# Reordered opening, moved addresses of x, and expert results scattered by token half in an attention + MoE kernel

## The reference

```
for t in range(S):                                    # attention, B=4 H=8 S=768 D=48
    y[t]  = r[t] @ (state + (u*k[t]) outer v[t])
    state = w * state + k[t] outer v[t]
h = x @ w_in;  x = (h * sigmoid(h)) @ w_out           # 384 -> 2048 -> 384
logits = x @ w_gate + modality_bias[modality_id]      # 8 experts
e = argmax(logits); p = softmax(logits)[e]
out = p * (relu(x @ w1[e]) @ w2[e])                   # 384 -> 1024 -> 384
```

## Time and profile before

| | us |
|---|---|
| three runs | 800.28, 800.82, 802.55; median 800.82 |
| profiled execution | 802.33, of which span 800.7 |
| PE busy | 748.7 (93%) |
| DVE, ACT, POOL busy | 503.0, 422.0, 228.3 |

### The profile page before, as it was taken

How to read it: one execution, slowest core, us unless ns; L and a number is a source line. 1 busy time by engine, 2 the same in 40 slices (tenths; PEclk the granted TensorE clock), 3 DMA queues, 4 the chain that set the end, 5 groups by cost and what they waited for, 6 DMA issues and landing times. The chain is left out here.

```text
span 800.7 us, 24974 instructions
## 1 busy us (share of the span) xinstructions
PE 748.7 (93%) x9894; PEld 728.6 (91%) x9894; DVE 503.0 (63%) x1349; ACT 422.0 (53%) x1076; POOL 228.3 (29%) x350
## 2 busy tenths in 40 slices
PE   3489999999999999999999999996989999999994
PEld 3478899999999999999999999996989999999994
DVE  7679765866576556656676657216856666556662
ACT  4476554545364545455554555435545665566552
POOL 4422221242224222322233212102415333323330
PEclk9599999999999999999999999998999999999998
DMA  8932221222222222122222210313576665665561
GB/s 318 377 134 74 63 99 53 88 73 95 74 95 74 94 76 93 57 82 69 95 74 94 75 58 2 118 82 118 193 163 239 235 234 197 227 248 213 213 223 55
DMA packets 24159, 104.94 MB, mean 131 GB/s; under 512 B 4411, under 2 KB 9800, under 8 KB 20482
## 3 DMA queue, kind: packets, MB, share of 16 engines
q1 hardware_dynamic: 19362, 93.34, 33.5%
q0 software_dynamic: 4704, 10.29, 3.8%
HBM read 93.90 MB, written 10.11 MB: 130 GB/s over the span
## 5 line engine op out<-in xcount | busy, mean ns | idle before, releaser
L635 ACT ACTIVATE g<-ps_h 128x256 f32<-128x256 f32 x192 | 73.9, 385 | 214.2 <-PE ps_h L1023 182.6
L1021 PE MATMUL ps_h<-x_hi,wi_hi 128*128 128x256 f32 x576 | 165.1, 287 | 8.5 <-DVE x_lo L806 7.7
L1022 PE MATMUL ps_h<-x_lo,wi_hi 128*128 128x256 f32 x576 | 162.7, 282 | 0.0
L1023 PE MATMUL ps_h<-x_hi,wi_lo 128*128 128x256 f32 x576 | 162.5, 282 | 0.0
L1038 PE MATMUL ps_o<-wo_hi,g_hi 128*128 128x392 f32 x384 | 135.4, 353 | 2.5 <-DVE g_lo L839 1.5
L1039 PE MATMUL ps_o<-wo_lo,g_hi 128*128 128x392 f32 x384 | 130.7, 340 | 0.0
L1040 PE MATMUL ps_o<-wo_hi,g_lo 128*128 128x392 f32 x384 | 130.4, 340 | 0.0
L839 DVE TENSOR_TENSOR g_lo<-g,g_hi 128x256 fp32r<-128x256 f32 x192 | 82.4, 432 | 71.2 <-ACT g_hi L628 69.3
L506 POOL TENSOR_TENSOR store<-store,up_half 128x256 f32<-128x256 f32 x44 | 33.8, 769 | 324.0 <-PE ps_y L1008 322.4
L1021 PEld LDWEIGHTS ps_h<-x_hi,wi_hi 128*128 128x128 f32 x576 | 108.9, 189 | 10.5 <-DVE x_lo L806 7.9
L1022 PEld LDWEIGHTS ps_h<-x_lo,wi_hi 128*128 128x128 f32 x576 | 109.1, 189 | 0.0
(11 more groups left out here) (199 smaller groups left out, 1528.3 us busy)
## 6 DMA issues: line engine op xcount, KB each, us to landing
store<-in_w SPq DMA_DIRECT2D x28, 1536.0 KB, 6.1
store<-in_quads SPq DMA_DIRECT2D x48, 704.0 KB, 4.7
x_rows<-rows SPq DMA_DIRECT2D x12, 384.0 KB, 3.1
woT_raw<-in_woT SPq DMA_DIRECT2D x4, 768.0 KB, 10.5
wi_raw<-in_wi SPq DMA_DIRECT2D x4, 768.0 KB, 10.3
wo_raw<-in_wo SPq DMA_DIRECT2D x4, 768.0 KB, 12.0
store<-x_rows,entries POOLq DMA_INDIRECT x26
out_rows<-y,entries_out POOLq DMA_INDIRECT x26
```

Of the source, the lines that this page charges most:

```text
L635: S.activation(g[:, F % 2, :], ps_h[F % 2][:, 0:ETOK], ACT.Silu).then_inc(g_made, 1)
L1021: T.matmul(out, hi, x_hi[:, t % 2, c, :], start=(c == 0), stop=False)
L1022: T.matmul(out, hi, x_lo[:, t % 2, c, :], start=False, stop=False)
L1023: last = T.matmul(out, lo, x_hi[:, t % 2, c, :], start=False, stop=(c == KC - 1))
```

## The change

In the opening: ACT does `first_states` right after `x_high(3)`, ahead of slot 0, and the splits of up chunks 4 and 5 too; in the slots the splits then run six ahead instead of four. DVE does `x_low(3)` ahead of `scale(4)` and `sum_bonus(4)`. An unused buffer of 336 fp32 words per partition stands ahead of `x_hi`, and `warm` moves behind `rows`; one of 248 words stands ahead of `xe_hi`. In the experts' block: PE does all down chunks of half 0, then those of half 1, with the turn at the same count of matmuls; ACT scales half 0 once `half_summed` says so, and half 1 at the end; POOL scatters each half on its own semaphore. Between tiles 1 and 2 POOL does `results_landed(1)` and `shift_entries(1)` ahead of the wait for the list entries. At the end SP waits for the landing of the results, and POOL does not.

```diff
@@ front_block, buffers
+        sb("x_place", [P, 336])
         x_hi = sb("x_hi", [P, 2, KC, ETOK], F32R)
         x_lo = sb("x_lo", [P, 2, KC, ETOK], F32R)
-        warm = sb("warm", [P, 4])
...
         rows = sb("rows", [P, 2, EB, W])
+        warm = sb("warm", [P, 4])
@@ ACT, opening and slots
             x_high(3)
+            first_states()
             wi_high(3)
+            wi_high(4)
+            wi_high(5)
...
-                if F == 0:
-                    first_states()
...
-                if F < FCH - 4:
-                    wi_high(F + 4)
+                if F < FCH - 6:
+                    wi_high(F + 6)
@@ DVE, opening and slots
             wi_low(2)
+            x_low(3)
             scale(4)
             sum_bonus(4)
-            x_low(3)
             wi_low(3)
+            wi_low(4)
+            wi_low(5)
...
-                if F < FCH - 4:
-                    wi_low(F + 4)
+                if F < FCH - 6:
+                    wi_low(F + 6)
@@ experts_block, buffers
+        sb("xe_place", [P, 248])
         xe_hi = sb("xe_hi", [P, KC, ETOK], F32R)
@@ SP, end
             sp.wait_ge(w2_in, 16 * tiles)
             sp.sem_inc(sp_passed, 1)
+            sp.wait_ge(y_out, 16 * EB * tiles)
+            sp.sem_inc(sp_passed, 1)
@@ POOL
             def results_out(j):
-                pool.wait_ge(y_made, j + 2)
-                pool.sem_inc(pool_passed, 1)
                 for i in range(EB):
+                    pool.wait_ge(y_half if i == 0 else y_made, j + 1 if i == 0 else j + 2)
+                    pool.sem_inc(pool_passed, 1)
...
+            results_landed(1)
+            shift_entries(1)
             tiles = tiles_with_tokens(pool)
             pool.wait_ge(listed, 16 * TB)
             load_entries(table, 3)
-            results_landed(1)
-            shift_entries(1)
...
             pool.wait_ge(entries_in, 16 * (tiles + 1))
-            results_landed(tiles)
+            pool.sem_inc(pool_passed, 1)
@@ ACT, end of a tile
                 x_high(j + 1)
+                act.wait_ge(half_summed, j + 1)
+                act.wait_ge(entries_kept, j + 1)
+                nc.scalar.activation(y[:, 0, :], ps_y[0][:, 0:DM], ACT.Copy, scale=entries_out[:, 0, 1:2].bitcast(F32)).then_inc(y_half, 1)
                 act.wait_ge(y_summed, j + 2)
-                act.wait_ge(entries_kept, j + 1)
-                for i in range(EB):
-                    last = nc.scalar.activation(y[:, i, :], ps_y[i][:, 0:DM], ACT.Copy, scale=entries_out[:, i, 1:2].bitcast(F32))
-                last.then_inc(y_made, 1)
+                nc.scalar.activation(y[:, 1, :], ps_y[1][:, 0:DM], ACT.Copy, scale=entries_out[:, 1, 1:2].bitcast(F32)).then_inc(y_made, 1)
@@ PE, down chunks
                 pe.wait_ge(y_made, j + 1)
-                for f in range(FCH):
-                    if f == (FCH - 2 if first else FCH // 2):
...
+                for i in range(EB):
+                    for f in range(FCH):
+                        if i == 1 and f == (FCH // 2 if first else 0):
...
-                last.then_inc(y_summed, 1)
+                    last.then_inc(half_summed if i == 0 else y_summed, 1)
```

More of the change, by code:

```diff
@@ L1179, in experts_block @@
         y_made = sem("y_made")
+        y_half = sem("y_half")
+        half_summed = sem("half_summed")
         y_out = sem("y_out")
@@ L1436, in tile @@
                 pe.wait_ge(y_made, j + 1)
-                for f in range(FCH):
-                    if f == (FCH - 2 if first else FCH // 2):
[L1439 to L1446, removed]
+                for i in range(EB):
+                    for f in range(FCH):
+                        if i == 1 and f == (FCH // 2 if first else 0):
+                            if first:
+                                pe.wait_ge(ranks_read, 1)
+                            pe.wait_ge(x_gathered, 16 * EB * (j + 1))
+                            turn()
+                        if i == 0:
+                            pe.wait_ge(h_lo_made, FCH * j + f + 1 + 4)
+                            if f % (FCH // PIECES) == 0:
+                                pe.wait_ge(w2_lo_made, PIECES * j + f // (FCH // PIECES) + 1)
                         hi, lo = (x[:, f, i * P:(i + 1) * P] for x in (h_hi, h_lo))
```

## The result

| | before | after |
|---|---|---|
| median of four runs, us | 800.55 (799.39 to 802.55) | 786.86 (786.45 to 787.36) |
| profiled execution, us | 802.33 | 786.88 |
| its span, us | 800.7 | 785.2 |
| PE busy, us | 748.7 | 742.9 |

The ratio is 0.9827, 95% interval 0.9806 to 0.9847: 13.7 us less, where 12.2 were forecast. The profiled execution of before lay 1.8 us above its median, so the two traces differ by more, 15.5 us.

A forecast was written before the change was run, and what follows sets the result against it. PE, busy 748.7 of 800.7 us, was taken as the bound: only its gaps and time per matmul count. Savings of 4.5 + 3.7 + 1.0 + 3.0 = 12.2 us gave 790.1 profiled, 788.6 median; range 780 to 796.

The forecast's parts named there:

- the likeliest case: Whole kernel: the forecast itself, all four terms come as summed, 788.6 us median; chance 0.43.
- Opening, 4.5 us: Opening: x_low(3) first, first_states and splits in ACT's idle time; 4.1 us plus half of an uncertain 0.8 saved.
- bounds of 2.5 and 6: Opening: 2.5 us saved if only the held-up x_low counts, nothing of DVE's idle time; 6 at most.
- The three moments named: Opening signs: PE's first up matmul at 33 us, slot 5's gate products near 49.4, DVE's 5.73 us gap gone.
- half of 0.8: Opening: splits done ahead leave DVE fewer wi_low pieces where it is full; half of an uncertain 0.8 us counted.
- Addresses, 3.7 us: Up matmuls: paddings shorten their spacing, dense to 117.8 ns (1.7 us), expert to 115.6 ns (2.0 us).
- POOL's order, 1.0 us: Expert tile 2: earlier copies remove PE's 2.43 us wait and half-speed stretch; 1.0 us saved, 3.7 saved to 1.5 lost.
- Late next is the gather: Expert tile 2: PE reaches the turn about 3.7 us earlier, near 604.3, and waits there for the gather instead.
- rival (e): SP's wait does not free POOL, and PE's wait for the gather costs a clock fall; 792.3 us, chance 0.04.
- `entries_kept` is made before: Expert tiles: ACT's new wait for half 0 holds up only its scaling, so halves cost nothing inside the tiles.
- Halves and SP's wait, 3.0 us: End: one activation and one scatter less, 1.8 us, and POOL's drain starting earlier, 1.2 us.
- rival (b): Up matmuls: addresses do nothing, 8.5 us saved in all, 792.3 us; chance 0.25.

The follow-up runs named there:

- e4_pool: Kernel before with only POOL's results_landed(1) and shift_entries(1) moved ahead of the wait for the list entries; 800.98 us, ratio 1.0010.
- e5_sp: Kernel before with only the end changed: SP waits for the landing of the results, POOL goes straight to its drain; 798.95 us, ratio 0.9983.
- e10_scan: Changed kernel with paddings of 368 and 312 words, plus 8 words ahead of g and 56 ahead of h_hi; 788.65 us.

## Why the prediction was right

786.86 us was measured, 788.6 forecast, and the likeliest case was the one that came. By the steps of the sum:

- **Opening, 4.5 us.** 5.1 measured alone, inside the bounds of 2.5 and 6. The three moments named came at 33.36 (33), 49.39 (near 49.4), and DVE's gap of 5.73 us shrank to 0.87 and 2.67, though it had been expected to go. Three details were off. The first product came 0.4 us later than the 32.95 of the sum, since x_low(3)'s three pieces took 2.30 us and not 1.95. DVE reached the end of `scale(4)` early enough for `scores` to follow the first up step at once (35.57), so the 0.7 us allowed for a wait there was not spent. And the splits ahead were worth 0.8 to 1.8 us, not half of 0.8.
- **Addresses, 3.7 us, called weakly founded.** 5.3 measured alone. That an address has a price, and the direction, came out as forecast, but not from the ground given: two speeds of one placement can't come from its address, and they recur in other traces with xe at 64. Each term was mis-sized: dense up gained 2.3 ns (1.0 taken), 3.9 us over 1728; expert up 0.8 (2.2 taken), 0.8 us over 936; and expert down 3.0 ns over 624 matmuls, 1.9 us, had no term. The prediction wrote that `h_hi` moves along, and asked no further. Dense down lost 0.3 ns, 0.3 us over 1152. That the part is off by no more than 1.6 us is luck: expert up was taken 1.2 us too large, the other two terms lacked 2.2 and 1.9.
- **POOL's order, 1.0 us.** Nothing: -0.8 alone, -0.2 between the changed kernel with the old and with the new order. This step failed. "Late next is the gather" was right, and the wait for it appeared, 1.10 us. The clock fall behind the wait, the price feared in rival (e), did not come: from 595.8 to 602.0 us the granted clock is 1.00,

```profile
595.80:602.00 6.20, 6.18 (x42) 6.19 (x43) 1.02 (x2) 0.86 (x2) 0.86 (x1) 1.00 0.89 317
```

and the half-speed stretch of before at this place is in none of the thirteen later traces, in each of which PE stands for about 1 us or more at one of these places, though for 2.03 us at most, where it stood 2.43 in before. What failed in the changed kernel is "`entries_kept` is made before", written of the halves inside the tiles: for tile 2's end it is made at 603, 5.62 us late, and costs PE 1.30 us ahead of tile 3. With the old halves (e4_pool) that wait is absent, and what ate the gain there stays open. The queue had to be followed one tile further, past `results_out(1)`, which the change left behind `gather(2)`.
- **Halves and SP's wait, 3.0 us.** 2.95 between the traces; 1.8 and 1.2 apart in theirs, as summed, and 2.2 and 1.4 by the ratios.

The sum of the parts measured alone, 5.1 + 5.3 + 2.2 - 0.8 + 1.4 = 13.2 us, stands beside 13.7 for all, so within the width of their intervals the parts add up. That the total came within 1.5 us of the 12.2 is partly luck: the addresses brought 1.6 us more than their term, and POOL's order 1.2 to 1.8 us less.

The rule weighed in the prediction, from the Trainium skill, SBUF — State Buffer, Who interferes with whom ("PE and ACT never wait on anyone"), would have given 792.3, rival (b). The runs show matmuls of one form at 116.35 to 119.26 ns by placement; the measurement decides against the reading that an address is free. Who waits for whom there no run shows. The dense down products, whose distance depends on how the offsets of `wo` and g go together, point to PE's own two reads.

## What to carry to other kernels

When a wait is taken away by reordering a queue, follow what is left behind the moved item by one more round: here a stall of the same size came back one tile later, and only issuing the finished scatters into POOL's idle time removed it. In a kernel bound by matmuls the start of each operand in SBUF is a parameter to be measured, by the distance of matmuls in one trace for each placement, for every tile that moves along too, and chunk by chunk where the other operand's start changes from chunk to chunk. A last step that takes a fixed time, such as POOL's drain, should start as early as possible, with another engine waiting for the data.

## What the runs showed of the hardware

- Matmuls of fp32r operands, 128 x 128 by 256 columns, follow each other at 116.35 to 119.26 ns on average by the offset of the moving tile. In the changed kernel's expert tiles single gaps run from 113 to 120 ns in a sequence that repeats. Matmuls of 384 columns take 173.5 to 174.0 or 175.9 to 176.5 ns by the offset of the stationary tile. Those of 392 columns in the dense stage take 178.0 to 178.6 on average, but 175.8 to 181.4 by chunk. A shift of 256 bytes left the expert up products' distances as they were; why 64 and 128 are bad for h and 0, 32, 96, 192 good stays open. The Trainium skill, TensorE: Matmul & The Clock Gate, Back-to-back issue gap, gives 262 cycles for 256 columns in a matmul by itself, from which 109 ns at 2.4 GHz are an estimate; no stretch of 24 gaps or more here averages under 113 ns.
- POOL's last drain needs 5.8 us with 70 transfers of its own in the block: from the end of its last issue where it waits for nothing (after, e5_sp), and from the landing where that is waited for first (before: 5.78 us, ending 7.0 us behind the last issue).
- How close to a large load a small transfer is issued decides when it lands. SP issues a weight load of 1536 KB at the turn in tile 2, in the changed kernel at

```profile
596.13 0.34 SPq L1204 DMA_DIRECT2D store<-in_w  x1
```

  and POOL's second scatter of tile 1's rows starts its issue at 595.65, 0.48 us ahead, is through with it at 596.67 and has landed only by 602.9, 6.8 us after the load's issue. In the five kernels with the full change (the changed kernel and the four placements) the scatter starts between 0.48 us ahead of the load and 0.38 behind it, and POOL then waits 5.7 to 6.5 us for it; in the seven kernels where it starts 1.35 us or more ahead, POOL waits 1.8 to 2.8 us. In the kernel before the scatter came 4.1 us behind a load (601.01, scatter 605.09), and POOL waited 2.3 us. So a scatter that is issued within half a microsecond of a weight load lands about when the load does: in e10_scan the load lands at 603.7 us and the scatter at 603.8. That is read from the traces side by side and was not varied by itself.
- The kernel before differs by 1.1 us at the start of tile 1 between executions (91.2 or 92.2 to 92.4) with no edit in the opening. The two early ones (e4_pool, e5_sp) have one more half-speed stretch of 3.4 us, from 54.0 and 53.4 us on, behind 2.0 us in which PE stood. With the new opening e10_scan alone has one (from 50.6, behind 1.78 us), and it too comes early, at 85.8 us where the others stand at 86.3 to 87.1. So a slower PE there does not cost its time at tile 1; why it comes with a gain stays open.
